# A three-pass gate on VectorE becomes clamp, square on ScalarE and maximum, and the keys are turned one slot earlier

## The reference

```python
k_p = k.reshape(B, H, Sp, 8, D).mean(axis=3)      # B 8, H 8, S 576, D 64
v_p = v.reshape(B, H, Sp, 8, D).mean(axis=3)
attn = softmax(q @ k_p^T / sqrt(D))
x = heads side by side of attn @ v_p              # 4608 x 512
h = x @ w_in;  g = where(h >= 1, h, where(h <= -1, 0, (h + 1)**2 / 4));  x = g @ w_out   # 512 -> 2048 -> 512
h = x @ w_in2; g = h * sigmoid(h);                                       out = g @ w_out2
```

## Time and profile before

| what | value |
|---|---|
| median of 3 runs | 1774.62 us (1773.8 to 1775.0) |
| profiled execution | 1774.56 us, of which the span is 1772.5 us |
| PE busy | 1690.7 us, 95% of the span |
| PE weight loads | 1364.2 us, 77% |
| DVE, ACT, POOL busy | 791.7, 424.9, 546.6 us |
| chain that ended last | PE 86%, DVE 8%, DMA 3%, issue 2%, ACT 2% |

### The profile page before, as it was taken

How to read it: one execution, slowest core, us unless ns; L and a number is a source line. 1 busy time by engine, 2 the same in 40 slices (tenths; PEclk the granted TensorE clock), 3 DMA queues, 4 the chain that set the end, 5 groups by cost and what they waited for, 6 DMA issues and landing times.

```text
span 1772.5 us, 20991 instructions
## 1 busy us (share of the span) xinstructions
PE 1690.7 (95%) x7568; PEld 1364.2 (77%) x7568; DVE 791.7 (45%) x1060; ACT 424.9 (24%) x712; POOL 546.6 (31%) x410
## 2 busy tenths in 40 slices
PE   5666899999999999999999999999999999999998
PEld 4455677777777777778888788888888888888887
DVE  3666685867667585865367412121211212121211
ACT  3222212212121212211123423222222222222222
POOL 4532253444435253442222222222222222222222
PEclk9888999999999999999999999999999999999999
DMA  5435344443525244441023301010101010101000
GB/s 137 98 77 135 108 103 115 93 107 78 128 66 121 85 103 114 88 112 59 0 66 99 121 0 48 1 47 0 47 0 47 0 47 3 45 12 35 17 6 24
DMA packets 139797, 114.96 MB, mean 65 GB/s; under 512 B 86676, under 2 KB 95892, under 8 KB 139764
## 3 DMA queue, kind: packets, MB, share of 16 engines
q1 hardware_dynamic: 139764, 114.53, 24.0%
HBM read 74.65 MB, written 39.85 MB: 65 GB/s over the span
## 4 chain that ended last, share of the span: by engine, by line
PE 86%; DVE 8%; DMA 3%; issue 2%; ACT 2%; SPq 0%; DVEq 0%; ACTq 0%
PE ps_y L585 14%; PE ps_y L586 14%; PE ps_y L587 14%; PE ps_h L585 14%; PE ps_h L587 13%; PE ps_h L586 13%; PE ps_a L555 1%; PE ps_a L526 1%; DVE g_tmp L968 1%; DVE g_tmp L966 1%; DVE g_tmp L971 1%; DVE prob L914 1%; DVE wout_lo L886 1%; DVE row_sum L907 1%; DMA y_dram<-y_sb 1%
## 5 line engine op out<-in xcount | busy, mean ns | idle before, releaser
L1047 POOL TENSOR_TENSOR g_lo<-g_tmp,g_hi 128x512 fp32r<-128x512 f32 x288 | 376.0, 1306 | 1146.9 <-ACT g_hi L790 1146.9
L585 PE MATMUL ps_h<-x_hi,win_hi 128*128 128x512 f32 x1144 | 454.7, 397 | 23.5 <-DVE x_lo L956 11.7
L587 PE MATMUL ps_h<-x_hi,win_lo 128*128 128x512 f32 x1144 | 448.4, 392 | 0.0
L586 PE MATMUL ps_h<-x_lo,win_hi 128*128 128x512 f32 x1144 | 448.3, 392 | 0.0
L975 DVE TENSOR_TENSOR g_tmp<-g_tmp,ps_h 128x512 f32<-128x512 f32 x144 | 99.1, 688 | 586.3 <-ACT g_tmp L786 586.3
L790 ACT ACTIVATE g_hi<-g_tmp 128x512 fp32r<-128x512 f32 x288 | 182.0, 632 | 641.3 <-DVE g_tmp L971 521.0
L585 PEld LDWEIGHTS ps_h<-x_hi,win_hi 128*128 128x128 f32 x1144 | 216.6, 189 | 87.0 <-issue 29.7
L587 PEld LDWEIGHTS ps_h<-x_hi,win_lo 128*128 128x128 f32 x1144 | 216.6, 189 | 45.9
L586 PEld LDWEIGHTS ps_h<-x_lo,win_hi 128*128 128x128 f32 x1144 | 216.8, 190 | 43.3
L585 PE MATMUL ps_y<-g_hi,wout_hi 128*128 128x512 f32 x576 | 229.1, 398 | 8.5 <-DVE g_tmp L971 7.2
L586 PE MATMUL ps_y<-g_lo,wout_hi 128*128 128x512 f32 x576 | 225.1, 391 | 0.0
(11 more groups left out here) (86 smaller groups left out, 1220.0 us busy)
## 6 DMA issues: line engine op xcount, KB each, us to landing
p_dram<-x_raw SPq DMA_DIRECT2D x28, 384.0 KB, 2.4
kv_raw<-in_k_dram SPq DMA_DIRECT2D x16, 576.0 KB
y_dram<-y_sb SPq DMA_DIRECT2D x36, 256.0 KB, 2.0
x_raw<-y_dram SPq DMA_DIRECT2D x18, 512.0 KB, 4.5
out_dram<-y_sb SPq DMA_DIRECT2D x36, 256.0 KB, 2.0
kv_raw<-in_v_dram SPq DMA_DIRECT2D x15, 576.0 KB
x_raw<-x_dram SPq DMA_DIRECT2D x16, 512.0 KB, 4.0
w_raw<-in_moe_w_in_dram SPq DMA_DIRECT2D x30, 256.0 KB, 3.8
```

What stands on the lines that cost most here:

```text
L585: mm(dst, w_h, a_h, start=first, stop=False)
L586: mm(dst, w_h, a_l, start=False, stop=False)
L587: return mm(dst, w_l, a_h, start=False, stop=last)
L1047: nc.gpsimd.tensor_tensor(g_lo[:, s % G_BUFS, :], g_tmp[:, s % T_BUFS, :], g_hi[:, s % G_BUFS, :].bitcast(F32), ALU.subtract).then_inc(g_l ...
```

## The change

The keys' K piece goes from slot 3 to slot 2. On PE the order of instructions stays the same, on ACT the two key copies of the loop move ahead of the copy to `g_hi` of slice 1.

The gate of layer 0 becomes: clamp h to [-1, 1] on DVE, (t + 1) squared on ACT in place, then on DVE the old last pass. On both engines the function is cut in two, and the slot "before" stands between them: on DVE between clamp and maximum, on ACT between the square (or layer 1's sigmoid) and the copy to `g_hi`. ACT's exponential of a slot "before" thereby comes ahead of the copy.

```diff
-PIECES = {3: [("Q", 0), ("K", 0)]}
+PIECES = {2: [("K", 0)], 3: [("Q", 0)]}
...
-                attention_slot(0, 3, UNITS)
+                attention_slot(0, 2, UNITS)
...
-            def gate_high(B, s, layer):
+            def gate_begin(B, s, layer):
                 t = g_tmp[:, s % T_BUFS, :]
                 if layer == 1:
...
                     nc.scalar.activation(t, ps_h[:, s % 2, :], ACT.Sigmoid).then_inc(sigmoid_done, 1)
+                else:
+                    act.wait_ge(ramp_done, B * FC + (s + 1))
+                    nc.scalar.activation(t, t, ACT.Square, bias=1.0).then_inc(square_done, 1)
+
+            def gate_high(B, s):
+                t = g_tmp[:, s % T_BUFS, :]
                 act.wait_ge(g_done, B * FC + (s + 1))
...
                     before, behind = slots_of(B, s)
+                    gate_begin(B, s, layer)
                     for slot in before:
-                        attention_slot(B, slot, units, "KV")
+                        attention_slot(B, slot, units)
                     if s == FC - 1 and more:
                         split_input(B + 1, 0)
-                    gate_high(B, s, layer)
+                    gate_high(B, s)
                     if s == FC - 1 and more:
                         split_input(B + 1, 1)
-                    for slot in before:
-                        attention_slot(B, slot, units, "S")
                     for slot in behind:
-                        attention_slot(B, slot, units, "KSV")
+                        attention_slot(B, slot, units)
...
+            def gate_begin(B, s):
+                dve.wait_ge(h_done, B * FC + (s + 1))
+                if s >= T_BUFS:
+                    dve.wait_ge(g_lo_done, B * FC + (s - 1))
+                t = g_tmp[:, s % T_BUFS, :]
+                nc.vector.tensor_scalar(t, bank_of(B, s), -1.0, 1.0, ALU.max, ALU.min
+                                        ).then_inc(ramp_done, 1)
+
+            def gate_end(B, s, layer):
+                h, t = bank_of(B, s), g_tmp[:, s % T_BUFS, :]
                 if layer == 0:
-                    nc.vector.tensor_scalar(t, h, 1.0, 1.0, ALU.min, ALU.add).then_inc(ramp_done, 1)
-                    dve.wait_ge(ramp_done, B * FC + (s + 1))
-                    nc.vector.scalar_tensor_tensor(out=t, in0=t, scalar=0.0, in1=t, op0=ALU.max,
-                                                   op1=ALU.mult).then_inc(square_done, 1)
                     dve.wait_ge(square_done, B * FC + (s + 1))
                     nc.vector.scalar_tensor_tensor(out=t, in0=t, scalar=0.25, in1=h, op0=ALU.mult,
                                                    op1=ALU.max).then_inc(g_done, 1)
...
-                    gate(B, s, layer)
                     before, behind = slots_of(B, s)
-                    for slot in before + behind:
+                    if layer == 0:
+                        gate_begin(B, s)
+                    for slot in before:
+                        attention_slot(B, slot, units)
+                    gate_end(B, s, layer)
+                    for slot in behind:
                         attention_slot(B, slot, units)
```

## The result

The changed kernel takes 1765.96 us (1762.9 to 1768.06, 5 runs) where the kernel before takes 1775.0 (1773.8 to 1777.14, 5 runs): ratio 0.9945 [0.993, 0.9959]. The medians lie 9.0 us apart. The profiled execution took 1764.43 us, its span 1762.5, which is 10.0 us less than before.

A forecast was written before the change was run, and what follows sets the result against it. PE bounds the loop, waiting only for copied keys; block 0 is bound by a ring of DVE, SP and ACT. Block 0's 8.5 us plus the loop's 4.5 took 13.0 off 1774.56: 1761.6 us, range 1756 to 1769.

The forecast's parts named there:

- A loop block: Layer-0 loop: PE starts the scores 0.75 us sooner per block, limited by the turned queries; 4.5 us over six blocks.
- (a): Block 0, slices 2 and 3: the second gate pass's stalls behind POOL go, PE's awaited maximum comes sooner; 2.2 us.
- (b): Block 0, slice 7: normalise and turn start sooner, but SP's next load also waits for POOL's pooling; 1.0 us.
- (c): Block 0, slice 9: unit 3's take comes sooner, but row_den and product meet POOL's pooling passes; 0.7 us.
- (d): Block 0, slice 12: normalise follows the clamp directly, row_den inherits POOL's pass, the turn is done sooner; 2.9 us.
- (e): Block 0, twelve matmuls after PE's 3.83 us idle: full clock instead of mostly 1.2 GHz; 1.7 us.
- More than that: Rival: port free for row_den everywhere, 6.7 us in the loop and 9.9 in block 0; 1758 us, chance 0.12.
- Gives back: Rival: DMA landings and POOL's order eat most of block 0's later gains; about 1767.5 us, chance 0.18.
- The slower rival: Rival: in loop blocks slice 8's bank is released late for hidden slice 10; 1781 us, chance 0.05.

The follow-up runs named there:

- e6_values_first: Changed kernel with ACT's copy of the attended values put ahead of the square in the slot before; 1763.6 us, ratio 0.9928.
- e9_order_bank: e4_order_only with one operand of the second DVE gate pass read from the PSUM bank instead of g_tmp; 1770.57 us, ratio 0.9959.
- e4_order_only: Changed kernel with the square given back to DVE, so new order and moved keys but three DVE passes; 1788.05 us, ratio 1.0068.
- e10_before_bank: Kernel before with one operand of its second gate pass read from the PSUM bank instead of g_tmp, nothing moved; 1772.35 us, ratio 0.9974.
- e2_gate_only: Changed kernel with the keys put back in slot 3, so only the new gate and its order; 1769.94 us, ratio 0.9957.
- e8_both: Changed kernel with the value copy ahead of the square and ten throw-away matmuls ahead of hidden slice 12 of block 0; 1761.54 us, ratio 0.9921.

## Why the prediction was nearly right, step by step

All places are counted from the first gate (65.70 before, 67.38 after), so that the first stretch drops out.

- **A loop block: right, row by row.** Forecast, as distance from the clamp's start: maximum's end 3.26, turn's start 6.40, queries' end 9.97, scores 10.01. Measured: 3.25, 6.36, 9.92, 10.05. The gap fell from 0.96 to 0.24. Row_den meets POOL's pass as expected and takes 1.12 us. Six blocks: 4.7 for 4.5, which is in part luck, since block 1 gave 1.3 us and the other five 0.67 each, for the 0.75 forecast. Also right is that the keys alone do as much.
- **(a): right.** PE's start of the outputs (81.17 in the earlier trace rows, now 80.62) comes 2.23 us sooner, for 2.2.
- **(b), (c): right only in sum.** L302 comes 3.9 us sooner (138.38 in the second profile of before, against 134.97 and now 132.76, shows that this place varies by 2 us), the turn of slice 9 5.2. But hidden slice 12, which should have gained the 3.9 of (a) to (c), gained 3.68: more was won in (b) and (c) than I gave them, and about 1.5 of it was lost again at the value copy behind the square (from the turn to hidden slice 12 it is 12.1 us, 10.6 before the change and 10.6 in e6_values_first). That hold-up isn't in the prediction at all, though the order of ACT's list shows it: I counted what the exponential and the keys gain there, not what the values lose.
- **(d): right.** From the clamp of slice 12 to the turn it is 3.89 us now, 6.55 before: 2.66, for 2.9. The clamp starts and row_den inherits POOL's pass:

```profile
171.69 0.69 DVE L973 TENSOR_SCALAR g_tmp<-ps_h 128x512 f32<-128x512 f32 x1
...
172.10 2.38 POOL L251 TENSOR_TENSOR kv_raw<-kv_raw 72x1024 f32<-72x1024 f32 x1 [2.32 <-DMA kv_raw<-in_k_dram]
...
173.06 1.45 DVE L914 TENSOR_SCALAR row_den<-row_sum 128x8 f32<-128x8 f32 x1
...
175.58 0.98 DVE L928 STREAM_TRANSPOSE x_raw<-prob 128x768 f32<-128x768 f32 x1
```

- **(e): the step that failed.** The gate that PE waited for at 189.50 now ends 6.5 us sooner (184.61), for 6.8; the matmuls behind ran at full clock, in 2.88 us instead of 4.61, for the 1.7 forecast. But I took them to be a cost of this wait, and priced them from the one profile of fourteen that shows them there. In the changed kernel the twelve that ran at the lower clock were those of hidden slice 12, 5.4 us instead of 3.0, and PE came to slice 15 only at 185.89, with no idle left: 5.3 us sooner, not 6.5. So (d) and (e) together came short by the 1.5 us that block 0 lacks (7.0 for 8.5). The kernel before pays 4.4 us at slice 12 in its second profile, so (e) should have been priced near zero. Nor is it shown why the changed kernel's twelve took 5.4 us in both its profiles, where most other kernels took 4.4 to 4.6 and only e9_order_bank 5.3.
- **The start.** In the sum the profiled execution was taken as the kernel's own; it was 1.3 us early up to the first gate compared with its second profile, whose execution took 1776.28 us. The medians of before in the later runs (1775.8 to 1776.4) lie 1.3 to 1.8 above the 1774.56 from which the sum was made. 11.7 below these would be 1764 to 1765. Of the 4.4 us between forecast and median, 1.3 are block 0 and the loop together (11.7 for 13.0), 1.7 the first stretch; the median of the five runs is a further 1.5 above the profiled execution, which the runs of before show as well (a range of 3 us).
- **The rivals.** "More than that" fell: row_den still waits for POOL (its 9.9 us for block 0 were never broken down). "Gives back" is the nearest in its number (1767.5) but not in its reason: (d) stood, and what was lost was the clock and the value copy. The slower rival did not occur, PE waits nowhere for slice 8's bank in the loop. Half of its reason was right for e4_order_only, the run that did get slower: the maximum comes late behind the turn. But what that held up was POOL's pooling and, behind it, SP's read-back, not a bank.
- **The two rules of the Trainium skill.** The Trainium skill, "ScalarE: Activation LUTs", section "What ACT_TABLE_LOAD costs", adds about 93 ns for a bias through a pointer. The square with its bias of 1.0 took 632 ns and the copy 631 (the rows of L789 and L796): the rows don't show that surcharge; they also don't show whether the 1.0 is read through a pointer. The Trainium skill, "SBUF — State Buffer", section "SBUF: two separate sides", has GpSimd and a DVE instruction with two SBUF inputs, or in a 2-port mode, lock each other out of the shared ports. By that rule an operand in PSUM frees the pass, and row_den waits if it runs in such a mode; the 0.69 of e10_before_bank, the 2.72 of e4_order_only and the 1.12 of row_den agree.

## What to carry to other kernels

Where one engine's passes stand still behind another's, as DVE's do here behind POOL's, count which instructions can be held and which of them the new order puts beside the other engine: with an operand in PSUM for the pass, row_den and the product stayed as they were in the old order and grew longer in the new one. A stalled pass in the new order cost 17.5 us that the same pass with a PSUM operand didn't. When an instruction is put in front of others in an engine's list, price every piece behind it, the ones that feed a DMA queue first. And take slow matmuls after an idle PE as a cost that wanders: look for it in several profiles before it is booked as a gain.

## What the runs showed of the hardware that I had not expected

- The length of PE's idle alone does not say how the twelve matmuls behind it run. After 3.11 us they took 3.0 us (before, slice 12), after 2.58 us 4.4 (second profile of before), after 2.49 us 3.0 (the same, slice 15), after 3.83 us 4.6, after 4.24 us 5.4, after 4.84 us 4.6 (e2_gate_only).
- POOL's last pooling pass (`v_sum`) was quicker in the changed kernel, with no change to POOL's code: a mean of 1028 ns from 208 to 807 us before and 735 after. It isn't that L968 is gone: in e4_order_only, which still has that pass and its stalls, the mean is 732, and in e10_before_bank, where the pass no longer stalls, 994. What in the order of DVE does it is not shown (groups by line: before, after, e4_order_only):

```profile
L251 POOL TENSOR_TENSOR v_sum<-kv_raw 72x256 f32<-72x256 f32 x12 | 12.3, 1028 | 0.0
```

```profile
L251 POOL TENSOR_TENSOR v_sum<-kv_raw 72x256 f32<-72x256 f32 x12 | 8.8, 735 | 0.0
```

```profile
L251 POOL TENSOR_TENSOR v_sum<-kv_raw 72x256 f32<-72x256 f32 x12 | 8.8, 732 | 0.0
```

- The first row_den of the kernel takes 0.17 us (e4_order_only) to 1.29 (the changed kernel). POOL's first pooling pass began at 9.70 us in the one and at 10.75 in the other, and row_den ends with POOL's pass in progress. Whether this sets the scatter of the first stretch is not shown: e10_before_bank has 0.29 there and its first gate at 67.91, e8_both 0.92 and 65.93.
